# A fused attention and two expert layers on one core: where the global distances are made, and when the first gathered rows are turned

## The reference

```python
# attention: q, k, v of 4 batches x 8 heads x 768 x 64, n_global = 8, n_local = 96
is_global = pos[None, :] < n_global
is_local = (rel >= 0) & (rel < n_local)
dist = np.where(is_global & ~is_local, n_local, np.abs(rel))
scores = q @ k.T / sqrt(64) - slope(head) * dist      # -1e9 where neither local nor global
out = softmax(scores) @ v
# experts 1: 3072 tokens x 512, 8 experts, 1024 hidden
e = argmax(x @ w_gate); gate = softmax(x @ w_gate)[e]; eom = sigmoid(x @ w_output_gate)[e]
x = gate * eom * (relu(x @ w1[e]) @ w2[e])
# experts 2: every expert takes at most 384 tokens, the highest logits first
x = relu(x @ w1[assigned]) @ w2[assigned]
```

## Time and profile before

| | us |
|---|---|
| median of 3 runs | 1019.37 |
| lowest and highest | 1019.15, 1020.68 |
| the profiled execution, its own time | 1021.17 |
| its span in the profile | 1019.1 |
| TensorE busy | 900.6 (88%) |
| VectorE busy | 666.7 (65%) |
| ScalarE busy | 451.2 (44%) |
| GpSimd busy | 278.6 (27%) |

### The profile page before, as it was taken

One profiled execution on the slowest core, in us unless ns is written; L12 is line 12 of the kernel. 1 busy time (PEld: TensorE's weight loads), 2 busy tenths in 40 slices (PEclk: granted clock), 3 DMA queues, 4 the chain that ended last, 5 costly groups with the idle time before them and its releaser, 6 DMA issues.

```text
span 1019.1 us, 21783 instructions
## 1 busy us (share of the span) xinstructions
PE 900.6 (88%) x6182; PEld 756.2 (74%) x6183; DVE 666.7 (65%) x1802; ACT 451.2 (44%) x984; POOL 278.6 (27%) x277
## 2 busy tenths in 40 slices
PE   5889999984799999999999996444799999999996
PEld 3777777773588888888888785333489899898985
DVE  5678888768576968878786777566454645364521
ACT  4778888856434353535535252000133434342410
POOL 2122332300233434443343434100203313321211
PEclk9899999997899999999999998555799999999998
DMA  9577767452351615425343334000225453635100
GB/s 217 110 164 164 170 160 173 96 197 84 116 207 42 216 46 203 161 87 189 114 155 121 127 113 141 26 2 1 64 99 211 128 204 123 226 114 193 63 32 32
DMA packets 148735, 129.69 MB, mean 127 GB/s; under 512 B 104476, under 2 KB 116916, under 8 KB 148532
## 3 DMA queue, kind: packets, MB, share of 16 engines
q1 hardware_dynamic: 137696, 99.68, 33.0%
q0 software_dynamic: 10784, 28.99, 8.7%
q10 hardware_dynamic: 180, 0.11, 0.0%
HBM read 107.91 MB, written 20.85 MB: 126 GB/s over the span
## 4 chain that ended last, share of the span: by engine, by line
PE 71%; DVE 9%; issue 7%; SPq 4%; DMA 4%; ACT 3%; DVEq 2%; ACTq 0%; POOL 0%; POOLq 0%
PE ps_o L1316 14%; PE ps_s L1293 14%; PE ps_o L1726 9%; PE ps_s L1710 7%; PE ps_pT L1710 7%; PE ps_s L1726 4%; PE ps_t L1904 2%; PE ps_pT L1304 2%; PE ps_o L526 2%; DMA qn<-in_q 2%; DVE product L1532 1%; PE ps_s L496 1%; SPq L2174 1%; ACT arena_p L842 1%; PE ps_pT L509 1%
## 5 line engine op out<-in xcount | busy, mean ns | idle before, releaser
L1316 PE MATMUL ps_o<-w_split_parts,hs 128*128 x696 | 166.6, 395 | 4.2 <-issue 3.7
L1293 PE MATMUL ps_s<-w_split_parts,xs 128*128 x696 | 165.5, 393 | 2.5 <-ACT xs L1401 1.5
L1316 PEld LDWEIGHTS ps_o<-w_split_parts,hs 128*128 128x128 f32 x696 | 128.5, 188 | 31.3 <-issue 5.2
L1532 DVE SCALAR_TENSOR_TENSOR product<-y_sb,wg_all 128x512 bf16<-128x512 f32 x224 | 145.7, 688 | 7.7 <-issue 2.8
L1293 PEld LDWEIGHTS ps_s<-w_split_parts,xs 128*128 128x128 f32 x696 | 128.5, 188 | 28.3 <-issue 2.9
L842 ACT ACTIVATE arena_p<-arena_p,min_s 128x256 f32<-128x256 f32 (+1 forms) x192 | 92.3, 484 | 27.1 <-DVE min_s L707 26.5
L1726 PE MATMUL ps_o<-w_split_parts,hs 128*128 128x512 f32 x384 | 94.5, 397 | 0.0
L1523 DVE TENSOR_TENSOR w_split_parts<-raw,w_split_parts 128x1024 f32 (+1 forms) x68 | 78.7, 1220 | 19.2 <-ACT w_split_parts L1420 18.0
L1726 PEld LDWEIGHTS ps_o<-w_split_parts,hs 128*128 128x128 f32 x384 | 70.2, 188 | 16.4 <-ACT hs L1762 2.9
L1409 ACT ACTIVATE hs<-ps_pT 128x512 fp32r<-128x512 f32 x58 | 31.6, 597 | 112.5 <-PE ps_pT L1304 112.5
L1808 DVE TENSOR_TENSOR w_split_parts<-raw,w_split_parts 128x1024 fp32r<-128x1024 f32 x56 | 68.6, 1224 | 19.2 <-ACT w_split_parts L1770 19.2
(11 more groups left out here) (316 smaller groups left out, 1735.8 us busy)
## 6 DMA issues: line engine op xcount, KB each, us to landing
raw<-in_moe_w SPq DMA_DIRECT2D x32, 2048.0 KB
kn<-in_k SPq DMA_DIRECT2D x32, 192.0 KB, 3.5
qn<-in_q SPq DMA_DIRECT2D x32, 192.0 KB, 3.5
vn<-in_v SPq DMA_DIRECT2D x32, 192.0 KB, 2.8
x_rows<-arena_x SPq DMA_DIRECT2D x96, 64.0 KB, 1.6
va<-in_v SPq DMA_DIRECT2D x32, 120.0 KB, 2.6
wg_rows<-in_moe_w_gate SPq DMA_DIRECT2D x1, 2048.0 KB, 7.3
va<-in_v SPq DMA_DIRECT2D x32, 40.0 KB, 2.6
```

The costliest lines, as they stand in the source:

```text
L1293: last = nc.tensor.matmul(ps_s[:, f, :], xs[:, a, c * P:(c + 1) * P], weights(par, w, cols), start=(n == 0), stop=(n == len(passes) - 1))
L1316: last = nc.tensor.matmul(ps_o[:, bank, :], hs[:, a, c * P:(c + 1) * P], weights(par, 2 + w, slice(c * DM, (c + 1) * DM)), start=(n == 0), ...
L1532: nc.vector.scalar_tensor_tensor(product[:, e % 2, :], y_sb[:], 1.0, wg_all[:, e, :], ALU.mult, ALU.mult, accum_out=log_now[:, e:e + 1])
```

## The change

In the attention's opening the four instructions of `global_far` leave VectorE. GpSimd executes them right after the branch, on tiles of their own (`in_g`, `out_g`, `far_g`), with a new semaphore `global_made`. VectorE goes from the local distances to the low parts and waits for `global_made` only before it puts the two kinds together. Eight dummy matmuls stand ahead of the first scores in place of ten. In the experts' opening seven dummies stand in place of ten, and TensorE turns the first gathered rows before it waits for the gates; it first waits for `puts_known`, since the turned rows overwrite the bank that the put table is read from. Lines behind the edits have higher numbers in the changed kernel.

```diff
--- before.py
+++ after.py
@@ -147,6 +147,7 @@
         STEPS_HELD = 4
         neg_b, probs_b, probsT_b = [arena_p[:, PART_P * a:PART_P * (a + 1)].rearrange("p (s h c) -> p s h c", s=STEPS_HELD, h=2)
                                     for a in range(3)]
+        in_g, out_g, far_g = [arena_p[:, PART_P + P * a:PART_P + P * (a + 1)] for a in range(3)]
         min_s = sb("min_s", [P, 2 * STEPS_HELD])
         sums = sb("sums", [P, 4, QT])
         sums_b = sums[:].rearrange("p g i -> p (g i)")
@@ -242,6 +243,7 @@
         lims_in = sem("lims_in")
         form_known = sem("form_known")
         far_made = sem("far_made")
+        global_made = sem("global_made")
         dense_rel = sem("dense_rel")
         qk_in = [sem("qk_in0"), sem("qk_in1")]
         v_in = [sem("v_in0"), sem("v_in1")]
@@ -559,7 +561,7 @@
 
             for g in range(3):
                 turn(0, 0, 0, g)
-            for n in range(10):
+            for n in range(8):
                 nc.tensor.matmul(ps_pT[:, 1, :], warm[:, 0:P], warm, start=True, stop=True)
             score(0, 0)
             two_pairs(0, True, False)
@@ -602,11 +604,12 @@
 
 
             local_far(far[:, P:3 * P], rel[:, 0:2 * P], tmp[:, 0:2 * P])
-            global_far(tmp[:, P:2 * P], key[:, 0:P], tmp[:, 0:P])
             low_parts()
-            nc.vector.tensor_copy(far[:, P + PREV:2 * P], tmp[:, P:P + GK])
-
-            done(nc.vector.tensor_tensor(far[:, 0:P], far[:, 2 * P:3 * P], tmp[:, P:2 * P], ALU.min))
+
+            dve.wait_ge(global_made, 4)
+            nc.vector.tensor_copy(far[:, P + PREV:2 * P], far_g[:, 0:GK])
+
+            done(nc.vector.tensor_tensor(far[:, 0:P], far[:, 2 * P:3 * P], far_g, ALU.min))
 
             for hh in range(2):
                 last = nc.vector.tensor_scalar(bias[:, 0, hh, 0:NB_FAST], far[:, 0:NB_FAST], slopes[:, 0, hh:hh + 1], MASKED,
@@ -892,6 +895,16 @@
                                allow_small_or_imprecise_dtypes=True)
                 nc.gpsimd.iota(key[:], [[1, S]], base=0, channel_multiplier=0,
                                allow_small_or_imprecise_dtypes=True).then_inc(dense_rel, 1)
+            else:
+
+                pool.wait_ge(consts, 3)
+                ng, nl = lims[:, 0:1], lims[:, 1:2]
+                nc.gpsimd.tensor_scalar(in_g, key[:, 0:P], ng, None, ALU.is_lt).then_inc(global_made, 1)
+                pool.wait_ge(global_made, 1)
+                nc.gpsimd.tensor_scalar(far_g, in_g, nl, None, ALU.mult).then_inc(global_made, 1)
+                nc.gpsimd.tensor_scalar(out_g, in_g, -FAR, FAR, ALU.mult, ALU.add).then_inc(global_made, 1)
+                pool.wait_ge(global_made, 3)
+                nc.gpsimd.tensor_tensor(far_g, far_g, out_g, ALU.add).then_inc(global_made, 1)
             pool.wait_ge(far_made, 1)
             if fast:
 
@@ -1367,9 +1380,10 @@
                     next_up(b)
                     tail(b + 1)
 
+            pe.wait_ge(puts_known, 1)
+            turn_x(0)
             pe.wait_ge(gate_made, 1)
             nc.tensor.transpose(ps_s[0:TILES, 2, 0:P], gate[:, 0:TILES], ident[:]).then_inc(gate_turned, 1)
-            turn_x(0)
             up(0)
             turn_x(1)
             turn_h(0)
@@ -2349,7 +2363,7 @@
                 nc.tensor.matmul(ps_o[:, 1, :], warm[:, 0:P], warm, start=True, stop=True)
             pe.wait_ge(consts, 4)
             by_form(pe, pe_banded, pe_dense, pe_first_route)
-            keep_busy(10)
+            keep_busy(7)
             pe_experts(pe)
             pe_routing2(pe)
             pe_experts2(pe)
```

## The result

The changed kernel takes 1025.22 us (median of 20 runs, 1018.96 to 1030.13), the kernel before 1019.77 us on the same chip (20 runs, 1017.9 to 1025.14). The ratio is 1.0051 with a 95% interval of 1.0037 to 1.0065: slower, by some 5 us. The forecast of 1019.2 us was wrong, and the range, which ended at 1021.4, did not hold the time. The profiled execution of the changed kernel took 1027.08 us, with a span of 1025.2.

What follows compares the result with a forecast made beforehand. TensorE was taken to carry 71% of the chain of waits, bound by the third pair's load and, at the experts, by its dummies. Terms of 0 and −0.17 us gave 1019.2 us from a 1019.37 median, range 1018.1 to 1021.4.

Steps and rivals of the forecast that it cites:

- Four instructions leave VectorE: Attention's opening: VectorE and first scores come 0.76 us earlier, swallowed by TensorE's two load waits; worth 0.
- The same four on GpSimd: Attention's opening: GpSimd has the global distances ready at 9.3 us by columns, so VectorE does not wait; worth 0.
- Ten dummies become eight: Attention's opening: eight dummies end near 11.6 us, ahead of scores that start at about 12.2; worth 0.
- Seven dummies at the experts: Experts' opening: with seven dummies and rows turned first, the gates' turn starts at 260.86 against 261.03; −0.17 us.
- so the rows are in: Experts' opening: transfers had sunk to 7 GB/s after 259.5, so the first gathered rows have landed and turn without waiting.
- The clock rival: Experts' opening: the clock is missed and the first product starts at 1.2 GHz; 2.3 us, giving 1021.5; chance 0.16.
- falls in it: Experts' opening, second form of the missed clock: the clock falls in TensorE's pause of about 2 us before the first product.
- a rise later than 261.0: Experts' opening: the point from which the missed clock was said to decide, a clock rise later than about 261.0 us.
- nothing but the gates' turn counts: Experts' opening: rows ready early move nothing, as ScalarE still copies gates and issues their store first; worth 0.
- the rule that I weighed: Experts' opening: a skill page says transposes do not count as busy for the clock in the same way, giving 1021.5.
- The sum: Whole kernel: every part worth 0 except −0.17 us at the experts' opening, so −0.17 us in all.
- slower: Whole kernel: slower by over 0.2%, above 1021.4 us; chance 0.10.

Runs made afterwards that it cites:

- e4: Kernel before with eight dummies instead of ten ahead of the first scores, nothing else: 1019.14 us, ratio 1.0012.
- e6: Kernel before with VectorE's low parts moved ahead of its global distances, none on GpSimd, ten dummies: 1020.99 us, ratio 0.9996.
- f4: Kernel before with low parts first, VectorE still making the global distances behind them and GpSimd making them too: 1019.57 us, ratio 1.0001.
- e3: Kernel before with the attention's part of the change but all ten dummies kept, experts' opening as before: 1021.35 us, ratio 1.0018 to before.
- e1: Kernel before with the attention's part of the change alone (GpSimd's global distances, eight dummies): 1023.14 us, ratio 1.0039.
- e7: Kernel before with GpSimd making the global distances too, unused, VectorE's order and work as before: 1019.91 us, ratio 0.9994.
- f1: Changed kernel plus 26 dummy matmuls ahead of the third pair's turns: 1018.73 us, ratio 0.9983 to the kernel before.
- e2: Kernel before with the experts' part of the change alone (seven dummies, first rows turned ahead of the gates): 1019.95 us, ratio 1.0002.
- e8: Changed kernel timed and profiled again, nothing altered: 1023.90 us, ratio 1.0038 to the kernel before.
- e9: Changed kernel with ten dummies again instead of seven at the experts' opening: 1024.71 us, ratio 1.0045 to the kernel before.
- g2: Kernel before with the experts' part of the change and 26 dummies ahead of the third pair's turns: 1017.03 us, ratio 0.9974.
- e10: Changed kernel plus eight dummies behind the gates' turn, in the pause before the first product: 1023.78 us, ratio 1.0031 to the kernel before.
- e11: Changed kernel plus eight dummies behind the gates' turn and 26 ahead of the third pair's turns: 1019.48 us, ratio 0.9994 to the kernel before.
- f3: Kernel before with the experts' part of the change, eight dummies behind the gates' turn and 26 ahead of the third pair's turns: 1016.64 us, ratio 0.9977.
- g1: Kernel before with the attention's part of the change (eight dummies included) and 26 dummies ahead of the third pair's turns: 1017.89 us, ratio 0.9983.
- f2: Kernel before plus only 26 dummies ahead of the third pair's turns: 1016.02 us, ratio 0.9967.

## Why the prediction was wrong, step by step

**Four instructions leave VectorE, worth 0.** The local steps came out: low parts at 10.08 (I said 9.96), scores 0.64 earlier (0.76), the gain swallowed by the two load waits. What failed is the conclusion that a gain which meets a wait is free. I looked at cover, whether VectorE was in time, and not at two other things that the edit moves. The pauses of TensorE get longer by what the work ahead of them is earlier (the second pair's by 0.74 us; the third pair's, without dummies in it, is 8.2 us on average in six profiles with the move and 6.8 in seven without), and the work behind them runs at the clock that it finds there. How long a pause is does not settle that clock: behind the second pair's it was 0.50 after 0.81 us in e4 and 1.00 after 1.52 in e6. And VectorE's later instructions stand four places further forward in its program, which changes where it waits for them in the loop. f4 (no cost with the four kept) against e3 and e1 speaks for their leaving as what costs, but e3's interval touches f4's and e1 has the eight dummies too; the 0.6 us in the loop is measured on the profiles. How the other 1.3 to 1.7 us, up to 60 us, arise is only argued: the fifth pair's pause and its clock are part of it. The cause of this half stays open: a program of VectorE padded to the old length, which would tell position from work, was not tried.

**The same four on GpSimd.** Right: 0.65, 0.75, 0.29 and 0.46 us, done at 9.35 where I had 9.3, and no wait. The two engines do slow each other. Timeline of VectorE in the kernel before, and then in the changed one:

```profile
6.90 0.35 DVE L580 TENSOR_SCALAR arena_p<-arena_x,lims 128x256 f32<-128x256 f32 x1 [1.05 <-issue]
7.08 0.48 DVE L582 TENSOR_SCALAR arena_p<-arena_x,lims 128x256 f32<-128x256 f32 x1 [1.05 <-issue]
9.03 0.59 DVE L586 TENSOR_TENSOR arena_b<-arena_b,arena_p 128x256 f32<-128x256 f32 x1
```

L582 took 0.48 us beside GpSimd's first instruction and 0.35 alone, L586 0.59 beside its fourth and 0.42 alone. The Trainium skill's page GPSIMD Engine Reference, section Specifications, says that the two contend when VectorE's instruction has two inputs in SBUF or runs in a two-port mode. GpSimd's second, beside two instructions of VectorE with two inputs (L583, L584), took 0.75, and its third, beside one with a single input (L585), 0.29, which fits; but the third takes its factors from the program and the second one from a tile, and the first took 0.65 mostly beside L582, which has a single input, so these rows do not prove it. GpSimd was not held until the end of VectorE's local part at 9.62, and e7, with no cost, shows that it doesn't matter here.

**Ten dummies become eight: worth 0.** Not refuted: e4's interval, 0.9991 to 1.0032, holds it. e1 and e3 differ by two dummies and by 2 us, with intervals that touch; that stays open. The profiles do show something there that I had no term for: from about 15.4 us the clock is at 0.50 for 3.4 us in six of the nine kernels with eight dummies and in two of the eleven with ten. The long wait for the third pair follows and can take that time up.

**Seven dummies at the experts, "so the rows are in": −0.17.** The net came out at 0.16, by luck. The gather took 3.99 us from issue to landing, so in the clock of the trace before its rows came at 256.05 + 3.99, 260.04, and not before 259.5: I took a stretch of idle DMA for the completion. TensorE waited 0.42 us for them. But by then the clock was up, and the gates' turn started 0.47 us behind the rows' turns and not 0.91.

**The clock rival, 0.16.** This was the mechanism at the experts, in the form that I named second, "falls in it", or rather at the start of the work behind it, and my 2.3 us stand against 1.6. The point from which I let it decide, a rise later than 261.0, was the wrong one: the clock rose ahead of the pause in every profile but f1's, where it was at 0.50 until well into the product. I had written that nothing but the gates' turn counts, and overlooked that the four turns had stood *inside* the pause before the first product. Moved ahead, they leave it empty: it was 1.52 us before and is 1.25 to 1.52 in the ten profiles with the old order and no dummies in it, and 1.86 in the six with the new one and none in it (the changed kernel, e2, e8, e9, f1, g2). In all six the product ran in part at 1.2 GHz, by a fall in five and in f1 by a clock that had not risen yet; in none of the ten did it, nor in e10, e11 and f3, whose new order has eight dummies in the pause. That the turns are transposes, on which the rule that I weighed rests, was not tested: in the changed kernel the clock was up before they began (1.00 at 265.2).

**The sum.** −0.17 was forecast and +5.4 measured. By the runs: 1.6 in the first product, less the 0.2 won there; 1.6 in the attention (g1 against f2), of which 0.6 in the loop; and 1.5 to 3.2 at the end of the experts' loop. That is 4.5 to 6.2. It counts too much by what comes back behind the first product: from its end to the first turns behind the loop's last wait (587.74 in the kernel before, 594.64 in the changed one) the two profiles of the changed kernel take 319.5 and 319.8 us, those of the kernel before 318.8 and 317.7. With this 0.7 to 2.1 in place of 1.5 to 3.2 the sum is 3.7 to 5.1. That also fits e2, whose slow product does not show in its time, and the 0.7 us of g2 against f2. The attention's 1.6 was taken with the 26 dummies; without them e3 and e1 have 1.8 and 3.9, so the sum closes only within the intervals. The loss at the end of the loop rests on two profiles with the fall against one, e9 (the changed kernel with three more dummies), that waited 1.45 us there without it and was no faster for that, at 1.0045 with 1.0023 to 1.0068 (e10 had no fall there either, at 1.0031); why the clock falls there in some and not in the kernel before, after as long a wait, was not settled. I gave "slower" 0.10, since I judged each half by one mechanism, and had no row in my list for what an edit does 300 us behind it.

## What to carry to other kernels

Before moving work out of a pause of TensorE, or ending the work ahead of one earlier, ask what the granted clock is on the far side: here a pause grown by 0.3 us made the product behind it slower by 1.6 us, ten times the 0.16 us that the move won, though half of that came back later. A long, unavoidable wait for a load may be worth filling with dummy matmuls up to just before the landing: 26 of them won 3.4 us of 1019, part of it perhaps elsewhere in the program. And an edit that adds or drops instructions ahead of a loop should be compared with one that keeps their number; waits marked "issue", counted in the two profiles, are a place to look when the work is the same and the time is not.

## What was not expected of the hardware

VectorE's waits marked "issue" inside a loop went with what stands ahead of the loop: 1.4 us in 7 waits or 2.7 in 12, by four instructions, in all twenty profiles. TensorE's wait at the end of the experts' loop was 1.15 to 2.82 us in every kernel without the 26 dummies, eight more matmuls in e10 left it at 1.16, and it is missing with the 26. So of the 3.4 us that these win in the kernel before, 1.2 to 2.2 may lie there and not at the third pair; dummies of the same number in another place were not tried. One GpSimd operation on 128 x 128 with factors from the program took 0.29 us, as long as VectorE's L588 on 128 x 128. And the first gather took 3.63 to 4.12 us from issue to landing in the six profiles that have it on the chain (3.99 in the changed kernel), although the DMA engines were 2% busy in the stretch in which it would land in the kernel before.
